# Moving the product of xs with at ahead of the product for n8 on TensorE

## The reference, cut to what matters

```python
for t in range(S):
    y[:, :, t] = np.einsum('bhd,bhde->bhe', rt, state)
    Sa = np.einsum('bhde,bhe->bhd', state, at)
    state_decay = state * wt[:, :, None, :] - np.einsum('bhd,bhe->bhde', Sa, bt)
    state = state_decay + np.einsum('bhd,bhe->bhde', vt, kt)
```

## Time and profile before

| what | value |
|---|---|
| median of 3 runs | 1015.53 us (1014.71 to 1015.89) |
| the profiled execution, its own time | 1013.78 us |
| its span in the trace | 1011.8 us |
| PE busy over the span | 958.3 us (95%) |
| DVE, ACT, POOL busy | 500.4, 349.0, 301.7 us |
| granted TensorE clock, mean | 0.988 |
| first stage (recurrence) | up to about 370 us |

### The profile page before, as it was taken

One profiled execution on the slowest core, in us unless ns is written; L12 is line 12 of the kernel. 1 busy time (PEld: TensorE's weight loads), 2 busy tenths in 40 slices (PEclk: granted clock), 3 DMA queues, 4 the chain that ended last, 5 costly groups with the idle time before them and its releaser, 6 DMA issues. The chain is left out here.

```text
span 1011.8 us, 48583 instructions
## 1 busy us (share of the span) xinstructions
PE 958.3 (95%) x21467; PEld 911.6 (90%) x21468; DVE 500.4 (49%) x941; ACT 349.0 (34%) x758; POOL 301.7 (30%) x361
## 2 busy tenths in 40 slices
PE   6899999999999679998999999999999999999995
PEld 4788988888888568888999999999999999999995
DVE  4366677766767356765444333346733223322330
ACT  3466666665665433332221111232322112211220
POOL 6456655565566417705200000027500000000000
PEclk9999999999999999999999999999999999999998
DMA  7256666676665344302000000003100000000000
GB/s 250 101 185 210 196 198 202 196 229 209 199 211 174 96 122 156 102 1 68 25 0 0 0 0 0 0 0 107 37 1 20 20 0 19 19 19 6 13 19 19
DMA packets 50249, 86.80 MB, mean 86 GB/s; under 512 B 6066, under 2 KB 29746, under 8 KB 50194
## 3 DMA queue, kind: packets, MB, share of 16 engines
q1 hardware_dynamic: 48578, 81.96, 25.5%
q0 software_dynamic: 880, 3.69, 1.2%
q10 hardware_dynamic: 736, 0.48, 0.2%
HBM read 70.37 MB, written 7.86 MB: 77 GB/s over the span
## 5 line engine op out<-in xcount | busy, mean ns | idle before, releaser
L1412 ACT ACTIVATE d_h_hi<-d_bank 128x384 fp32r<-128x384 f32 x96 | 47.1, 491 | 200.1 <-PE d_bank L1494 200.1
L1449 DVE SCALAR_TENSOR_TENSOR d_h_lo<-d_bank,d_h_hi 128x384 fp32r<-128x384 f32 x96 | 53.5, 558 | 78.1 <-ACT d_h_hi L1412 78.1
L1508 PE MATMUL d_bank<-w_lo,d_h_hi 128*128 128x320 f32 x288 | 89.0, 309 | 0.0
L1508 PE MATMUL d_bank<-w_hi,d_h_lo 128*128 128x320 f32 x288 | 89.0, 309 | 0.0
L1508 PE MATMUL d_bank<-w_hi,d_h_hi 128*128 128x320 f32 x288 | 89.0, 309 | 0.0
L1412 ACT ACTIVATE c_h_hi<-c_bank 128x384 fp32r<-128x384 f32 x80 | 37.5, 489 | 146.4 <-PE c_bank L1494 146.4
L1508 PE MATMUL c_bank<-w_hi,c_h_hi 128*128 128x320 f32 x240 | 74.8, 312 | 0.0
L1508 PE MATMUL c_bank<-w_hi,c_h_lo 128*128 128x320 f32 x240 | 74.1, 309 | 0.0
L1508 PE MATMUL c_bank<-w_lo,c_h_hi 128*128 128x320 f32 x240 | 74.1, 309 | 0.0
L1461 DVE TENSOR_TENSOR d_o<-d_bank,u_all 128x320 f32<-128x320 f32 x24 | 11.8, 492 | 111.0 <-PE d_bank L1508 111.0
L1449 DVE SCALAR_TENSOR_TENSOR c_h_lo<-c_bank,c_h_hi 128x384 fp32r<-128x384 f32 x80 | 42.3, 554 | 40.9 <-ACT c_h_hi L1412 40.9
(11 more groups left out here) (265 smaller groups left out, 2792.1 us busy)
## 6 DMA issues: line engine op xcount, KB each, us to landing
e_raw<-in_e SPq DMA_DIRECT2D x72, 256.0 KB, 4.3
r_raw<-in_c SPq DMA_DIRECT2D x24, 768.0 KB, 4.3
tok<-tok_of SPq DMA_DIRECT2D x24, 320.0 KB, 2.7
e_raw<-in_e SPq DMA_DIRECT2D x24, 260.5 KB, 4.1
va<-in_c SPq DMA_DIRECT2D x24, 160.0 KB, 2.5
vb<-in_c SPq DMA_DIRECT2D x24, 160.0 KB, 2.7
attention_out<-yout SPq DMA_DIRECT2D x92, 40.0 KB, 2.0
stage<-in_moe_w_ch POOLq DMA_DIRECT2D x4, 640.0 KB, 6.9
```

Source lines behind the costliest of these rows:

```text
L1412: nc.scalar.activation(h_hi[:, m, :], bank[m % 4][:, 0:TW], ACT.Relu).then_inc(h_hi_done, 1)
L1449: nc.vector.scalar_tensor_tensor(h_lo[:, m, :], bank[m % 4][:, 0:TW], 0.0, h_hi[:, m, :].bitcast(F32), ALU.max, ALU.subtract).then_inc(h_l ...
L1508: last = nc.tensor.matmul(bank[4 + t % 2][:, 0:E], lhs, rhs, start=(m == 0 and i == 0), stop=(m == NM - 1 and i == 2))
```

## The change

In TensorE's list n8 and rhs_a change places, and so do their blocks in the code that is unrolled into the loop. No other list, wait, semaphore, bank or tile is touched. TensorE's order is then m2, rhs_v, rhs_a, n8, ut, tokk, m3.

```diff
-            ("n4", -1), ("upd_k", -3), ("upd_b", -3), ("n4t", -1), ("sol3", -2), ("xsd", -2), ("m2", -1), ("rhs_v", -1), ("n8", -1),
-            ("rhs_a", -1), ("ut", -2), ("tokk", 0), ("m3", -1)]
+            ("n4", -1), ("upd_k", -3), ("upd_b", -3), ("n4t", -1), ("sol3", -2), ("xsd", -2), ("m2", -1), ("rhs_v", -1), ("rhs_a", -1),
+            ("n8", -1), ("ut", -2), ("tokk", 0), ("m3", -1)]
...
                 last.then_inc(ready["rhs_v"], 1)
-            if name == "n8":
-                take(n, "xsd", -1)
-                for j, par in halves:
-                    q = tok_half(par)
-                    last = mm(out[q, j * C:j * C + C], nt[2][q, j, :], nn[2][q, j, :])
-                    took(n, 2 * j + par, last, ("xsd", -1))
-                last.then_inc(filled["n8"], 1)
             if name == "rhs_a":
                 take(n, "xs")
                 take(n, "rhs_v")
...
                 last.then_inc(filled["rhs_a"], 1)
+            if name == "n8":
+                take(n, "xsd", -1)
+                for j, par in halves:
+                    q = tok_half(par)
+                    last = mm(out[q, j * C:j * C + C], nt[2][q, j, :], nn[2][q, j, :])
+                    took(n, 2 * j + par, last, ("xsd", -1))
+                last.then_inc(filled["n8"], 1)
```

## The result

The kernel after took 1031.12 us (median of 4 runs, 1027.64 to 1031.78) against 1015.12 us, a ratio of 1.0152 with a 95% interval of 1.0126 to 1.0179. One more execution of that kernel took 1344.49 us at a granted clock of 0.651, and one of the kernel before (e5) 1069.61 us at 0.839; these two are in no ratio here. The kernel after is slower by 10 to 16 us; forecast were 11.7 us and 1027.2 us.

A forecast was written before the change was run, and what follows sets the result against it. TensorE's own work plus its short gaps was taken to bound the kernel. 22 turns at 0.53 us add 11.7 us to 1015.53, giving 1027.2 us, 1.15% slower; range 1019.0 to 1031.5 us.

The forecast's parts named there:

- tokk is held by the addition: TensorE's tokk loads wait for DVE's n8 addition, starting 0.11 us after it ends; after the change 0.53 us later.
- The wait of rhs_a for rhs_v: TensorE's wait for its own rhs_v matmuls, no longer covered by n8: 0.11 us after their end, costing 0.33.
- The bound below, 0: Lower bound on the uncovered rhs_v wait's cost: nothing, if the semaphore is up in time; upper bound 0.47 us.
- n8 and the addition: n8 starts 0.47 us after rhs_a, 0.8 later than before; DVE's addition starts 0.05 after n8's matmuls and takes 0.68.
- The 0.3 us that n8 had to spare: Slack of n8's matmuls before the change, because DVE was still busy with m2's addition; some 0.3 us.
- m3 to abk: TensorE's step from m3's to abk's loads at the loop's end, taken as 0.47 us, making abk 0.53 late.
- the reading from the loop's first turn: The branch needs the m3-to-abk time, as in the first turn, where abk began 0.49 us behind m3, 0.28 idle.
- the hidden branch: Rival: only POOL's at holds abk behind m3; abk 0.27 us late, 5.9 us in all, 1021.5 us, chance 0.20.
- How often: Groups 1 to 22 pay 0.53 us in 22 loop turns, 11.7 us; first and last groups taken as 0.
- Dearer: Rival: n8 starts 0.12 us later and TensorE's own wait costs 0.14 more; 0.79 a turn, 1032.9 us, chance 0.09.
- No change: Rival: TensorE's own wait is free and the branch hidden; within 0.2% of 1015.53 us, chance 0.10 including a 1019.9 variant.
- Faster: Rival: rhs_a and POOL's at come sooner, tokk not waiting for the addition; 0.24 us a turn, 1010.2 us, chance 0.04.

The follow-up runs named there:

- e5: The kernel before, unchanged, run and traced a second time; ratio 1.0001 to before, turn 13.235 us.
- e2: Kernel after, with n8 written into the first bank of m3's pair and the wait for its addition moved from tokk to m3; ratio 1.0003 to before.
- e9: Kernel before, with n8 written into the first bank of m3's pair so tokk need not wait for the addition; ratio 1.0004 to before.
- e10: Kernel after, with the order rhs_v, m2, rhs_a, n8 and n8 in m3's bank; 1011.17 us, ratio 0.9961 to before.
- e11: Kernel after, with the order rhs_v, m2, rhs_a, n8, n8 in m3's bank and the loop cut behind abk; ratio 0.9984 to before.
- e1: Kernel before, same order, with TensorE's wait for its own rhs_v put ahead of n8 instead of rhs_a; ratio 1.0047 to before.
- e4: Kernel after, same TensorE sequence, with the loop's branch moved from ahead of abk to between abk and sol0; ratio 1.0093 to before.
- e8: Kernel before, with n8 and rhs_a exchanged only for the last group, in the unrolled end; ratio 1.0008 to before.
- e3: Kernel after, with the order changed to rhs_v, m2, rhs_a, n8; ratio 1.0069 to before, turn 13.603 us.

## Why the prediction was right

*tokk is held by the addition.* Right. tokk began 0.11 to 0.12 behind the addition's end in every kernel that kept the wait (0.12 in after), and the gap went in e2, e9, e10 and e11.

*The wait of rhs_a for rhs_v.* Right, at 0.37 against the 0.33 taken: rhs_a began 0.84 behind rhs_v, 0.15 after rhs_v's matmuls ended, where I took 0.11. The bound below, 0, fell with the trace of after and with e1. The Trainium skill's figure (TensorE: Matmul & The Clock Gate, Single matmul latency), which the page gives for a single bf16 matmul over the full array and which would have made it 0.18, was too small for these fp32 matmuls of 64x64.

*n8 and the addition.* The steps of 0.47 and 0.05 measured 0.46 and 0.04, and the addition took 0.69 where 0.68 was taken. The 0.3 us that n8 had to spare went as reckoned; DVE stood 0.49 before the addition.

*m3 to abk.* The choice between the two readings decided half of the price (0.53 or 0.27). POOL's at ended 0.71 before abk (328.55 against 329.26) and the step was 0.46 all the same, so the reading from the loop's first turn was right and the hidden branch wrong. e4 put 0.34 of the step on the loop's end. The row of the first turn was the only support for it, so the choice was a judgement that came out, not a thing known. The 108 ns of the Trainium skill (Advanced Engine Details and Errata, Control Flow Timing) is a third of what shows on TensorE here.

*How often.* 22 turns at 0.588 give 12.9 where the forecast was 11.7 (12.7, since the second turn pays 0.37 only: from its rhs_v to the next it took 13.44 before and 13.81 after, and in before it has no gap at tokk but is 0.22 longer than a steady turn). 0.04 of the 0.058 more a turn are the longer wait for itself. What the change does beyond its turns was taken as 0, and e8 bears that out for the last group to 2.6 us (1.0008, up to 1.0026). Whether the first group pays nothing can't be read: in the trace of after the clock was at its lower level just there (0.50 from 34 to 38 us).

What the prediction lacked was the scatter: it took 2 us as what runs of this kernel can tell apart. The two measurements of the kernel after, four runs and five, differ by 4.9 us in the median (1031.12 and 1026.21), with 1027.2 forecast between them. That the forecast is nearly the second one, and that the first still lies in the range, 0.4 us inside its upper end of 1031.5, is luck in part: 12.7 us are explained by turns, and the other 3 of the first measurement, or the 2 less in the second, are not. Where the clock falls around the loop is the likely cause, but it is not shown run by run.

*Rivals.* "Dearer" was wrong for the turn (0.588, not 0.79). "No change" would have needed both a free wait and a hidden branch. "Faster" needed tokk not to wait; with that wait taken away (e2) the turn was still 0.1 longer than before, since rhs_a gets no earlier by being put first (0.85 behind rhs_v) and n8 and ut get later.

## What to carry to other kernels

Before a unit is moved ahead of another, ask what the other was covering: here n8 hid TensorE's wait for its own matmuls (0.37 us), and the move bought nothing for it, since rhs_a started at 0.84 behind rhs_v in either order. A unit whose result is drained by a busy engine has slack only until that engine is free; past it every further delay went straight to tokk here, which waits for the same bank, and another bank (e2) gave back 0.48 of the 0.59 us where another order (e3) gave back 0.20. Read a short change from the period of the loop, not from two spans: its mean repeated to 0.02 us where the times of one kernel differed by several us. But a difference of a few hundredths in it is no more certain than one in the spans.

## What the runs showed that I had not expected

- The end of TensorE's loop, its branch, costs 0.34 us behind a unit of 16 short loads and still 0.25 us behind one of 64 (e4).
- A unit of 16 bf16 loads that begins after an idle stretch lets the next unit begin 0.22 us later (e1: 305.00 to 305.22), against 0.37 behind a running fp32 unit; so a part of an uncovered wait comes back. m2 and rhs_v behind the same idle time are 0.25 apart (after: 325.32 to 325.57).
- m3 follows tokk after 0.64 us where tokk's transposes ran on from ut's, and after 0.59 where tokk had waited (e2, e9, e10 against after).
- TensorE's loads start 0.15 us after its own last matmul's end when they wait for it, a little more than the 0.11 to 0.13 after DVE's or POOL's.
